# GLA attention fused with two MLPs on one core: the states' part of y in a bank of its own, the copy of k behind the sigmoid, and a new order of loads

## The chip, the cores and the metric

The kernel runs on one core of a Trainium2 chip. TensorE (PE) multiplies matrices and writes to PSUM, VectorE (DVE), ScalarE (ACT) and GpSimd (POOL) work on elements, SyncE (SP) only issues DMAs. Each engine works through its own instructions in the order in which they are written and waits at semaphores. The metric is the device time in microseconds of one execution. Times differ from run to run; a difference of 2% is what a measurement of this kernel can tell from no change.

## The reference, cut to what matters

```python
# attention: q, k, v, f_logit are (4, 8, 768, 48)
f = 1.0 / (1.0 + np.exp(-f_logit))
for t in range(S):
    state = f[:, :, t, :, None] * state + np.einsum('bhd,bhe->bhde', k[:, :, t], v[:, :, t])
    y[:, :, t] = np.einsum('bhd,bhde->bhe', q[:, :, t], state)
# x = y as (3072 tokens, 384)
gate = 1.0 / (1.0 + np.exp(-(x @ w_gate)))       # first MLP, d_ff 1536
x = gate * (x @ w_val) @ w_out
h = x @ w_in                                     # second MLP, d_ff 2048
out = (h * (1.0 / (1.0 + np.exp(-1.702 * h)))) @ w_out2
```

## The kernel before

**Attention.** A unit is a pair of heads and 256 tokens, 48 units in all, four to a step of 256 tokens (three steps to a batch, so that every third step begins with an empty state: `third` is 0). ACT turns f_logit into decays (`forget`, L545 and L546), DVE scans them (L722), takes the reciprocal (L726) and keeps the last value of each chunk (L727); the three together are `prepare`. POOL multiplies q and k by them (`decay`: q_dec L474, k_dec L479). The buffers f_raw, q_raw and k_raw have two slots, so that the loads for unit n must wait until unit n-2 was used: on SP, `load_kq(n)` waits for q_dec and then for k_dec of unit n-2.

**Visits.** PE does the matmuls of attention in 53 visits. The list `VISITS` says of each which unit is turned, kept and made; from the tenth on, visit n has (n, n-1, n-2). `turned`: two transposes of k_dec into the bank turn_ps (L914), which ACT copies to k_rows (`take_k`, L564), and the scores k_dec x q_dec (L957), which DVE masks (L734). `kept`: k_rows x v (L947), from which DVE makes four new states (L744, then a chain of three or four L752). `made`: scores x v (L935), and on top of these sums in the same columns the states times q_dec (L968), which make y. ACT copies y out (`take_y`, L570), and SP moves it by two or three small DMAs into x_raw, the input of the first MLP (`move_y`, L369).

**The MLPs.** Each product is made of three matmuls in a reduced format (L975 to L977: high x high, low x high, high x low), so that every operand is split into x_hi/x_lo, w_hi/w_lo and act_hi/act_lo. The first MLP goes through seven groups of tokens (two of 256, five of 512; here group 0 to 6) and in each through 12 blocks of hidden columns, j = 0 to 11. A block is on PE: 9 matmuls for the gate, 9 for the value (`hidden`), at some j a visit, then 9 matmuls of the block before into out_ps (`out`). ACT makes the sigmoid (L634) and act_hi (L640), DVE the product (L823) and act_lo (L832). The gate's matmuls of the next block wait for the sigmoid of this one, the value's for the product. Visits 0 to 7 run ahead of the MLP. Group 0 has visits at five blocks, groups 1 to 5 at j = 0, 1, 3, 4, 5, 7, 8 and 9. In group 0 DVE also splits the first MLP's weights (w_lo, L776), whose loads and high parts are ACT's (L520, L526).

**Where groups meet.** At j = 10 ACT makes the three slabs of x_hi for the next group (`x_first_part`, L584), and DVE then x_lo (L769). Slab k of x_hi needs the moved y of the first k+2 units of the next group's last step, so that the third slab needs the y that was made in this group's last visit, at j = 9. At j = 10 DVE also prepares the unit one further than the visit at j = 9 turned; PREPARE_AT sets this.

**SP's order.** For each visit SP issued the moves of y, v, then q and k for the unit three ahead, then f for the unit four ahead:

```python
if made is not None:
    move_y(made)
    load_v(made + 4)
if turned is not None:
    load_kq(turned + 3)
    load_f(turned + 4)
```

Of the kernel before, what the change touches and what calls it, by code (L numbers as in the profile page):

```python
# [12 lines left out]
P = 128  # L13
# [3 lines left out]
def gla_moe_moe2(nc, q_t, k_t, f_t, v_n, v_t, w1, w2, out_t, x_dram, x2_dram):  # L17
# [52 lines left out]
    for g in range(NG1 - 1):  # L70
        if g == 0:
            forgets = {j: n + 3 for n, j in enumerate((1, 2, 4, 6, 8))}
            prepares = {j: n + 1 for n, j in enumerate((0, 1, 3, 5, 7, 9))}
        else:
            forgets = {j: n + 3 for n, j in enumerate((0, 1, 3, 4, 5, 7, 8, 11))}
            prepares = {j: n + 2 for n, j in enumerate((0, 2, 3, 4, 6, 7, 10, 11))}
        FORGET_AT.update({(g, j): ahead_of + n for j, n in forgets.items()})
        PREPARE_AT.update({(g, j): ahead_of + n for j, n in prepares.items()})
        ahead_of += len(forgets)
# [4 lines left out]
    with ExitStack() as ctx:  # L84
# [40 lines left out]
        state = sb("state", [P, 2, UG, CH, D])  # L125
        p_end = sb("p_end", [P, UNITS, CH])
# [6 lines left out]

# [23 lines left out]
        tiles_done = sem("tiles_done")  # L157
# [4 lines left out]
        y_taken = sem("y_taken")  # L162
# [172 lines left out]
        with nc.Block() as block:  # L335

            @block.sync
            def _(sp):
# [25 lines left out]
                def move_y(n, pieces=slice(None)):  # L364
                    u = Unit(n)
                    sp.wait_ge(y_taken, n + 1)
# [36 lines left out]
                move_y(3, slice(1, None))  # L403
                for n in range(4, 8):
                    load_v(n)
# [4 lines left out]
                for q in range(BLOCKS1):  # L410
# [41 lines left out]
            def _(pool):  # L452
# [13 lines left out]
                def decay(n):  # L466
# [5 lines left out]
                    if n >= 4:  # L472
                        pool.wait_ge(visit_done, out_visit[n - 4] + 1)
# [41 lines left out]
            def _(act):  # L515
# [33 lines left out]
                def first_move_y(n, pieces):  # L549
                    u = Unit(n)  # L550
                    act.wait_ge(y_taken, n + 1)
# [52 lines left out]
                take_y(0)  # L604
# [4 lines left out]
                take_y(1)  # L609
                first_load_f(6)  # L610
                forget(5)
                w1_first_part(1)
                take_y(2)
                first_move_y(2, slice(2, None))
                take_y(3)
                first_move_y(3, slice(0, 1))
                first_load_f(7)
                load_w1(2)
                take_k(4)
                x_first_part(0)  # L620
                load_w1(3)
                w1_first_part(2)
                load_w1(4)
                forget(6)
                forget(7)

                for q, b in enumerate(BLOCK):
# [13 lines left out]
                    if b.first_mlp and (b.g, b.j) in VISIT_AT:  # L641
                        turned, _, made = VISITS[VISIT_AT[b.g, b.j]]
# [62 lines left out]
            def _(dve):  # L705
# [7 lines left out]
                for ps in (att_ps, out_ps):  # L713
                    dve.memset(ps[:, 0:2, Y_COL:Y_COL + BLOCKS * C], 0.0).then_inc(gaps_set, 1)

                def prepare(n):
                    if n >= UNITS:
                        return
# [4 lines left out]
                                           ALU.max).then_inc(scan_done, 1)  # L723
                    dve.wait_ge(scan_done, n + 1)
# [3 lines left out]
                                    prod[:, u.s, :].rearrange("p (c t) -> p c t", c=CH)[:, :, C - 1]).then_inc(p_end_done, 1)  # L728

# [368 lines left out]
```

## Time and profile before

| | |
|---|---|
| Time, three runs | 968.01, 969.16 and 1051.86 us; median 969.16 us |
| Profiled execution | 968.01 us, its span 966.2 us |
| Busy | PE 98%, PE's weight loads 82%, DVE 51%, ACT 31%, POOL 11% of the span |
| Chain that ended last | PE 90%, DVE 4%, waits without a cause shown 2%, DMA 1%, SP's queue 1%, ACT 1% |
| Granted PE clock | 0.99 on average; half (1.2 GHz instead of 2.4) in two stretches before 40 us |

The slowest of the three times is of a disturbed run and is left out of comparisons. Three stages follow one another: up to about 34 us attention's first visits and the first loads; up to about 480 us the first MLP with visits between its blocks (group 0 to 79.6 us, group 1 to 137 us); then MLP work without visits. The busy time of PE is that of pipelined instructions that overlap, so it does not say that PE never waited; the start times of neighbouring rows do.

### The profile page before, as it was taken

What the parts mean: (1) busy time and instruction counts of PE and PEld (TensorE: products, weight loads), DVE (VectorE), ACT (ScalarE), POOL (GpSimd) and SP (SyncE); (2) the same over time, 40 slices, a digit from 0 to 9 for tenths busy, and PEclk for the clock granted to TensorE, in tenths of its full rate; (3) what the DMA queues carried; (4) which work ended last, traced back from release to release, by engine and by line L of the source; (5) the groups of instructions that cost most, each with busy time, mean ns of one, the idle gap of its engine ahead of it and who ended that gap; (6) DMA issues with size and microseconds to landing.
All of it is one profiled execution on the core that took longest, in us unless ns stands there. A gap on an engine that the chain in (4) does not pass through costs nothing.

```text
span 966.2 us, 17729 instructions
## 1 busy us (share of the span) xinstructions
PE 948.8 (98%) x7159; PEld 789.7 (82%) x7159; DVE 491.9 (51%) x876; ACT 303.7 (31%) x621; POOL 106.9 (11%) x125
## 2 busy tenths in 40 slices
PE   8899999999999999999999999999999999999997
PEld 5799988888888888888788888888888888888886
DVE  8897876547555664565333234344343443443433
ACT  3453332223222222322224333323332233333322
POOL 4211211101110111111003440000000000000000
PEclk9899999999999999999999999999999999999999
DMA  5652322112111211121022330020020100100000
GB/s 152 204 167 61 83 63 67 53 51 66 52 46 42 82 45 50 33 76 28 24 104 66 98 115 1 0 66 1 1 66 1 55 12 1 66 1 1 33 1 35
DMA packets 44005, 52.33 MB, mean 54 GB/s; under 512 B 8464, under 2 KB 33808, under 8 KB 43920
## 3 DMA queue, kind: packets, MB, share of 16 engines
q1 hardware_dynamic: 41056, 43.20, 15.4%
q10 hardware_dynamic: 2864, 7.95, 2.8%
q8 instruction: 59, 0.97, 0.4%
q14 instruction: 26, 0.21, 0.1%
HBM read 36.96 MB, written 9.44 MB: 48 GB/s over the span
## 4 chain that ended last, share of the span: by engine, by line
PE 90%; DVE 4%; issue 2%; DMA 1%; SPq 1%; ACT 1%; ACTq 0%; POOL 0%; DVEq 0%
PE up_ps L975 16%; PE up_ps L977 16%; PE up_ps L976 16%; PE out_ps L975 12%; PE out_ps L977 11%; PE out_ps L976 11%; PE att_ps L968 3%; PE att_ps L935 2%; PE att_ps L957 1%; DMA stage<-w 1%; PE turn_ps L914 1%; PE att_ps L947 1%; DVE w_lo L776 1%; DMA k_raw<-k_t 1%; DVE act_lo L832 0%
## 5 line engine op out<-in xcount | busy, mean ns | idle before, releaser
L975 PE MATMUL up_ps<-x_hi,w_hi 128*128 128x512 f32 (+1 forms) x792 | 294.2, 372 | 3.6 <-ACT act_f L634 3.0
L977 PE MATMUL up_ps<-x_hi,w_lo 128*128 128x512 f32 (+1 forms) x792 | 293.8, 371 | 0.0
L976 PE MATMUL up_ps<-x_lo,w_hi 128*128 128x512 f32 (+1 forms) x792 | 293.7, 371 | 0.0
L975 PE MATMUL out_ps<-act_hi,w_hi 128*128 128x512 f32 (+1 forms) x540 | 207.9, 385 | 0.7 <-DVE act_lo L832 0.7
L977 PE MATMUL out_ps<-act_hi,w_lo 128*128 128x512 f32 (+1 forms) x540 | 202.9, 376 | 0.0
L976 PE MATMUL out_ps<-act_lo,w_hi 128*128 128x512 f32 (+1 forms) x540 | 202.6, 375 | 0.0
L640 ACT CAST act_hi<-act_f 128x512 fp32r<-128x512 f32 (+1 forms) x180 | 106.5, 592 | 253.0 <-DVE act_f L823 180.7
L832 DVE TENSOR_TENSOR act_lo<-act_f,act_hi 128x512 fp32r<-128x512 f32 (+1 forms) x180 | 118.1, 656 | 113.7 <-ACT act_hi L640 113.7
L975 PEld LDWEIGHTS up_ps<-x_hi,w_hi 128*128 128x128 f32 x792 | 150.0, 189 | 30.0 <-issue 3.6
L976 PEld LDWEIGHTS up_ps<-x_lo,w_hi 128*128 128x128 f32 x792 | 150.1, 190 | 25.3
L977 PEld LDWEIGHTS up_ps<-x_hi,w_lo 128*128 128x128 f32 x792 | 150.1, 189 | 25.2
L826 DVE TENSOR_TENSOR act_f<-act_f,up_ps 128x512 f32<-128x512 f32 x96 | 66.0, 687 | 173.4 <-ACT act_f L636 173.4
L823 DVE TENSOR_TENSOR act_f<-act_f,up_ps 128x512 f32<-128x512 f32 (+1 forms) x84 | 51.1, 608 | 163.0 <-PE up_ps L977 159.5
L975 PEld LDWEIGHTS out_ps<-act_hi,w_hi 128*128 128x128 f32 x540 | 101.6, 188 | 22.2 <-DVE act_lo L832 1.2
L636 ACT ACTIVATE act_f<-up_ps 128x512 f32<-128x512 f32 x96 | 57.4, 598 | 192.9 <-PE up_ps L977 192.9
L977 PEld LDWEIGHTS out_ps<-act_hi,w_lo 128*128 128x128 f32 x540 | 101.6, 188 | 18.7
L976 PEld LDWEIGHTS out_ps<-act_lo,w_hi 128*128 128x128 f32 x540 | 101.7, 188 | 17.3
L634 ACT ACTIVATE act_f<-up_ps 128x512 f32<-128x512 f32 (+1 forms) x84 | 45.0, 535 | 176.8 <-PE up_ps L977 176.8
L726 DVE RECIPROCAL inv_prod<-prod 128x256 f32<-128x256 f32 x48 | 84.1, 1753 | 1.7
L474 POOL TENSOR_TENSOR q_dec<-q_raw,prod 128x256 f32<-128x256 f32 x48 | 35.2, 734 | 317.5 <-DVE prod L722 263.6
L752 DVE SCALAR_TENSOR_TENSOR state<-state,p_end 128x48 f32<-128x48 f32 x176 | 47.4, 269 | 6.2
L479 POOL TENSOR_TENSOR k_dec<-k_raw,inv_prod 128x256 f32<-128x256 f32 x48 | 37.8, 788 | 50.1 <-issue 41.0
(68 smaller groups left out, 511.7 us busy)
## 6 DMA issues: line engine op xcount, KB each, us to landing
stage<-w SPq DMA_DIRECT2D x16, 384.0 KB, 3.2
stage<-w ACTq DMA_DIRECT2D x9, 576.0 KB, 4.4
q_raw<-q_t SPq DMA_DIRECT2D x96, 48.0 KB, 1.9
k_raw<-k_t SPq DMA_DIRECT2D x96, 48.0 KB, 1.9
v_raw<-v_n SPq DMA_DIRECT2D x48, 96.0 KB, 2.2
x_raw<-x_dram SPq DMA_DIRECT2D x6, 768.0 KB, 4.5
out_t<-final SPq DMA_DIRECT2D x18, 256.0 KB, 2.3
f_raw<-f_t SPq DMA_DIRECT2D x80, 48.0 KB, 1.9
```

The costliest lines, as they stand in the source:

```text
L479: pool.tensor_tensor(k_dec[:, u.s, :], k_raw[:, u.s, :], inv_prod[:, u.s, :], ALU.mult).then_inc(k_dec_done, 1)
L634: act.activation(act_f[:, b.t, 0:b.n], up_ps[:, 0, 0:b.n], ACT.Sigmoid).then_inc(sig_done, 1)
L636: act.activation(act_f[:, b.t, 0:b.n], up_ps[:, b.j % 2, 0:b.n], ACT.Sigmoid, scale=1.702).then_inc(sig_done, 1)
L640: act.copy(act_hi[:, b.t, 0:b.n], act_f[:, b.t, 0:b.n]).then_inc(act_hi_done, 1)
L726: dve.reciprocal(inv_prod[:, u.s, :], prod[:, u.s, :]).then_inc(inv_done, 1)
L752: dve.scalar_tensor_tensor(out=after[:, c, :], in0=state_before(u, c), scalar=p_end[:, n, c:c + 1], in1=after[:, c, :], op0=ALU.mult, op1= ...
L823: dve.tensor_tensor(act_f[:, b.t, 0:b.n], act_f[:, b.t, 0:b.n], up_ps[:, 1, 0:b.n], ALU.mult).then_inc(mul_done, 1)
L826: dve.tensor_tensor(act_f[:, b.t, 0:b.n], act_f[:, b.t, 0:b.n], up_ps[:, b.j % 2, 0:b.n], ALU.mult).then_inc(mul_done, 1)
L832: dve.tensor_tensor(act_lo[:, b.t, 0:b.n], act_f[:, b.t, 0:b.n], act_hi[:, b.t, 0:b.n].bitcast(F32), ALU.subtract).then_inc(act_split, 1)
L975: pe.matmul(dst, w_hi[:, at:at + P], m_hi, start=first, stop=False)
L976: pe.matmul(dst, w_hi[:, at:at + P], m_lo, start=False, stop=False)
L977: return pe.matmul(dst, w_lo[:, at:at + P], m_hi, start=False, stop=last)
```

## The change

It has five parts.

1. The states' part of y no longer adds to the columns of scores x v. `from_states` writes it into the upper half of turn_ps, behind the visit's other matmuls. ACT copies it to y_t (`begin_y`), and DVE adds the part from the visit's bank (`make_y`), which makes y. For a unit that begins with an empty state, `from_states` multiplies a zero tile for the first chunk too, two matmuls more.
2. Within the visit the wait for the visit's own earlier matmuls (`tiles_done`) is gone; there are waits for ACT's copy of the k just turned (`k_rows_done`) and for the y part before (`y_begun`) in front of it, since all three use the bank turn_ps.
3. ACT copies k to k_rows between sigmoid and act_hi instead of behind act_hi.
4. SP issues f, q and k for the units ahead in front of the moves of y and of v.
5. Ahead of the MLP the orders differ: ACT issues the loads of the first weights and makes their high parts at other places, `forget(7)` moves into block 0, DVE splits unit 4's `prepare` around two visits, and it now handles the visits 5 and 6 as well.

```diff
-            forgets = {j: n + 3 for n, j in enumerate((1, 2, 4, 6, 8))}
+            forgets = {j: n + 2 for n, j in enumerate((0, 1, 2, 4, 6, 8))}
@@ SP, at each visit
+                        if turned is not None:
+                            load_f(turned + 4)
+                            load_kq(turned + 3)
                         if made is not None:
                             move_y(made)
                             load_v(made + 4)
-                        if turned is not None:
-                            load_kq(turned + 3)
-                            load_f(turned + 4)
@@ POOL, decay
-                    if n >= 4:
-                        pool.wait_ge(visit_done, out_visit[n - 4] + 1)
+                    wait(pool, states_used, n - 3)
@@ ACT
-                def take_y(n):
-                    u = Unit(n)
-                    act.wait_ge(visit_done, out_visit[n] + 1)
+                def begin_y(n):
+                    act.wait_ge(states_used, n + 1)
                     wait(act, y_moved[n % YS], 16 * moves(n % YS, n))
-                    act.copy(y_t[:, n % YS, :].rearrange("p (c r t) -> p c r t", c=BLOCKS, r=SIDES),
-                             banks(out_visit[n])[:, :, Y_COL:Y_COL + BLOCKS * C].rearrange("p r (c t) -> p c r t", c=BLOCKS)).then_inc(y_taken, 1)
+                    act.copy(y_t[:, n % YS, :], turn_ps[:, W:2 * W]).then_inc(y_begun, 1)
@@ ACT, ahead of the blocks (after)
+                begin_y(1)
+                first_load_f(6)
+                load_w1(2)
+                forget(5)
+                begin_y(2)
+                first_move_y(2, slice(2, None))
+                w1_first_part(1)
+                begin_y(3)
+                first_move_y(3, slice(0, 1))
+                w1_first_part(2)
+                load_w1(3)
+                take_k(4)
+                x_first_part(0)
+                load_w1(4)
+                forget(6)
@@ ACT, in a block
+                    turned = made = None
+                    if b.first_mlp and (b.g, b.j) in VISIT_AT:
+                        turned, _, made = VISITS[VISIT_AT[b.g, b.j]]
+                    if turned is not None:
+                        take_k(turned)
                     act.wait_ge(mul_done, q + 1)
                     wait(act, act_used, q - 1)
                     act.copy(act_hi[:, b.t, 0:b.n], act_f[:, b.t, 0:b.n]).then_inc(act_hi_done, 1)
-                        if turned is not None:
-                            take_k(turned)
-                        if made is not None:
-                            take_y(made)
+                    if made is not None:
+                        begin_y(made)
@@ DVE
+                def make_y(n, v):
+                    dve.wait_ge(y_begun, n + 1)
+                    y = y_t[:, n % YS, :].rearrange("p (c r t) -> p r c t", c=BLOCKS, r=SIDES)
+                    own = banks(v)[:, :, Y_COL:Y_COL + BLOCKS * C].rearrange("p r (c t) -> p r c t", c=BLOCKS)
+                    dve.tensor_tensor(y, y, own, ALU.add).then_inc(y_done, 1)
@@ DVE, after_visit
-                    if made is not None:
-                        dve.wait_ge(y_taken, made + 1)
                     if turned is not None:
                         mask(turned, v)
                     if kept is not None:
                         new_states(kept, v)
+                    if made is not None:
+                        make_y(made, v)
@@ PE
+                def from_states(n, v):
+                    u = Unit(n)
+                    pe.wait_ge(state_done, states_before(n + 1))
+                    pe.wait_ge(k_rows_done, len([a for a, _, _ in VISITS[:v + 1] if a is not None]))
+                    wait(pe, y_begun, n)
+                    for c in range(CH):
+                        before = state_before(u, c) if u.third or c else no_state[:, :]
+                        for i in range(PAIR):
+                            last = pe.matmul(turn_ps[rows[i], W + c * C:W + (c + 1) * C], before[rows[i], :],
+                                             q_dec[rows[i], n % 4, c * C:(c + 1) * C], start=True, stop=True)
+                    last.then_inc(states_used, 1)
@@ PE, visit
+                    last.then_inc(visit_done, 1)
                     if made is not None:
-                        last.then_inc(tiles_done, 1)
-                        pe.wait_ge(tiles_done, made + 1)
-                        pe.wait_ge(state_done, states_before(made + 1))
-                        for c in range(0 if m.third else 1, CH):
-                            at = slice(Y_COL + c // SIDES * C, Y_COL + (c // SIDES + 1) * C)
-                            for i in range(PAIR):
-                                last = pe.matmul(ps[rows[i], c % SIDES, at], state_before(m, c)[rows[i], :],
-                                                 q_dec[rows[i], made % 4, c * C:(c + 1) * C], start=False, stop=False,
-                                                 skip_group_check=True)
-                    last.then_inc(visit_done, 1)
+                        from_states(made, v)
```

On SP, for the visit at j = 9 of group 1 (unit 15 made, unit 17 turned), before: two moves of y, v, q and k for unit 20, f for unit 21.

```order
L369 DMA x_raw<-y_t 48x256 [waits x_split,y_taken]
L369 DMA x_raw<-y_t 48x256
L361 DMA v_raw<-v_n 128x192 [waits visit_done]
L351 DMA q_raw<-q_t 48x256 [waits q_dec_done]
L351 DMA q_raw<-q_t 48x256
L354 DMA k_raw<-k_t 48x256 [waits k_dec_done]
L354 DMA k_raw<-k_t 48x256
L344 DMA f_raw<-f_t 48x256 [waits gate_done]
L344 DMA f_raw<-f_t 48x256
```

The same visit in the changed kernel: the two moves of y now stand behind the loads of q and k with their two waits.

```order
L345 DMA f_raw<-f_t 48x256 [waits gate_done]
L345 DMA f_raw<-f_t 48x256
L352 DMA q_raw<-q_t 48x256 [waits q_dec_done]
L352 DMA q_raw<-q_t 48x256
L355 DMA k_raw<-k_t 48x256 [waits k_dec_done]
L355 DMA k_raw<-k_t 48x256
L370 DMA x_raw<-y_t 48x256 [waits x_split,y_done]
L370 DMA x_raw<-y_t 48x256
L362 DMA v_raw<-v_n 128x192 [waits visit_done]
```

On PE, a visit of group 0 behind its transposes (block j = 2, unit 4 made), before.

```order
L957 MATMUL att_ps<-q_dec,k_dec 64x64 [waits q_dec_done]
L957 MATMUL att_ps<-q_dec,k_dec 64x64 x7
L968 MATMUL att_ps<-q_dec,state 48x64 [waits state_done,tiles_done]
L968 MATMUL att_ps<-q_dec,state 48x64 x7
```

The same place in the changed kernel: the eight matmuls of the states go to turn_ps, without the wait for the visit's own matmuls and with two others.

```order
L986 MATMUL att_ps<-q_dec,k_dec 64x64 [waits q_dec_done]
L986 MATMUL att_ps<-q_dec,k_dec 64x64 x7
L931 MATMUL turn_ps<-q_dec,state 48x64 [waits y_begun,k_rows_done,state_done]
L931 MATMUL turn_ps<-q_dec,state 48x64 x7
```

## Rows read from the trace of the kernel before

**Rows 1.** Busy time by stage (us, busy and count, PEclk, DMA share, GB/s).

```profile
34.00:79.60 45.60, 44.89 (x577) 42.73 (x577) 44.66 (x79) 21.26 (x48) 8.31 (x12) 0.93 0.54 157
79.60:137.00 57.40, 56.41 (x856) 53.11 (x857) 42.60 (x98) 20.22 (x62) 11.02 (x15) 1.00 0.28 74
```

**Rows 2.** The same view around the second stretch at half clock.

```profile
26.34:33.16 6.82, 4.41 (x46) 3.78 (x45) 3.79 (x7) 2.73 (x7) 2.99 (x4) 1.00 0.95 284
33.16:39.99 6.83, 5.90 (x53) 5.48 (x54) 5.97 (x8) 3.82 (x13) 1.46 (x2) 0.50 0.80 234
39.99:46.80 6.81, 6.72 (x107) 6.34 (x107) 6.64 (x13) 2.78 (x8) 1.47 (x2) 1.00 0.45 124
```

**Rows 3.** Who waited for whom (total us, times, longest): 138 to 480, DVE 34 to 79.6.

```profile
PEld att_ps L968 <- PE att_ps L957: 6.8, 30, 0.2
...
DVE act_f L823 <- ACT act_f L634: 2.0, 1, 2.0
```

**Rows 4.** Timeline of a visit in group 3, three chunks of states (start us, us).

```profile
238.05 0.38 PE L914 MATMUL turn_ps<-ident,k_dec 128*128 128x128 f32 x2
238.62 0.40 PE L947 MATMUL att_ps<-v_raw,k_rows 64*64 64x48 f32 x16
238.84 0.43 PE L957 MATMUL att_ps<-q_dec,k_dec 48*64 48x64 f32 x16
...
239.35 0.39 PEld L968 LDWEIGHTS att_ps<-q_dec,state 48*48 48x48 f32 x12 [0.23 <-PE att_ps L957]
...
239.82 0.19 PEld L975 LDWEIGHTS out_ps<-act_hi,w_hi 128*128 128x128 f32 x1
```

**Rows 5.** Timeline, weight loads of a visit with four chunks of states.

```profile
142.50 0.50 PEld L968 LDWEIGHTS att_ps<-q_dec,state 48*48 48x48 f32 x16 [0.23 <-PE att_ps L957]
143.09 0.19 PEld L975 LDWEIGHTS out_ps<-act_hi,w_hi 128*128 128x128 f32 x1
```

**Rows 6.** Timeline of the first visit: transposes and ACT's copy of k.

```profile
8.85 0.38 PE L914 MATMUL turn_ps<-ident,k_dec 128*128 128x128 f32 x2
...
9.27 0.37 ACT L564 COPY k_rows<-turn_ps 128x256 f32<-128x256 f32 x1 [3.40 <-PE turn_ps L914]
```

**Rows 7.** Timeline of DVE in group 0.

```profile
55.91 0.41 DVE L734 TENSOR_TENSOR scores<-att_ps,causal 128x256 f32<-128x256 f32 x1
...
56.24 0.34 DVE L744 TENSOR_TENSOR state<-att_ps,p_end 128x192 f32<-128x192 f32 x1
```

**Rows 8.** Timeline, end of the stage before the blocks.

```profile
31.72 1.15 ACT L526 CAST w_hi<-stage 128x1152 fp32r<-128x1152 f32 x1 [2.99 <-DMA stage<-w]
...
33.59 0.36 ACT L634 ACTIVATE act_f<-up_ps 128x256 f32<-128x256 f32 x1
...
33.98 0.42 DVE L823 TENSOR_TENSOR act_f<-act_f,up_ps 128x256 f32<-128x256 f32 x1 [2.01 <-ACT act_f L634]
```

**Rows 9.** Timeline of SP's queue, end of group 2.

```profile
212.01 1.98 SPq L369 DMA_DIRECT2D x_raw<-y_t  x2
...
223.72 0.78 SPq L354 DMA_DIRECT2D k_raw<-k_t  x2
```

**Rows 10.** Timeline of ACT and PE, end of group 2.

```profile
219.28 1.66 ACT L584 CAST x_hi<-x_raw 128x512 fp32r<-128x512 f32 x3
222.05 0.60 ACT L634 ACTIVATE act_f<-up_ps 128x512 f32<-128x512 f32 x1 [1.10 <-PE up_ps L977]
...
225.93 0.39 PE L975 MATMUL up_ps<-x_hi,w_hi 128*128 128x512 f32 x1
```

**Rows 11.** Timeline of SP's queue and PE, end of group 1.

```profile
137.06 0.78 SPq L354 DMA_DIRECT2D k_raw<-k_t  x2
...
136.59 0.47 PE L975 MATMUL up_ps<-x_hi,w_hi 128*128 128x512 f32 x1 [0.26 <-DVE x_lo L769]
...
137.63 0.49 PE L975 MATMUL up_ps<-x_hi,w_hi 128*128 128x512 f32 x1
```

**Rows 12.** DMA issues (count, KB each, median us to landing).

```profile
x_raw<-y_t SPq DMA_DIRECT2D x71, 48.0 KB, 2.0
```

More of the change, by code:

```diff
@@ L78, in gla_moe_moe2 @@
         PREPARE_AT.update({(g, j): ahead_of + n for j, n in prepares.items()})
-        ahead_of += len(forgets)
+        ahead_of += 5 if g == 0 else 8
     SPLIT_AT1 = 10
@@ L125, in gla_moe_moe2 @@
         state = sb("state", [P, 2, UG, CH, D])
+        no_state = sb("no_state", [P, D])
         p_end = sb("p_end", [P, UNITS, CH])
@@ L156, in gla_moe_moe2 @@
         k_rows_done = sem("k_rows_done")
-        tiles_done = sem("tiles_done")
         visit_done = sem("visit_done")
@@ L161, in gla_moe_moe2 @@
         state_done = sem("state_done")
-        y_taken = sem("y_taken")
+        states_used = sem("states_used")
+        y_begun = sem("y_begun")
+        y_done = sem("y_done")
         y_moved = sems("y_moved", YS)
@@ L365, in move_y @@
                     u = Unit(n)
-                    sp.wait_ge(y_taken, n + 1)
+                    sp.wait_ge(y_done, n + 1)
                     wait(sp, x_split, u.group * KC)
@@ L403, in _ @@
                 move_y(3, slice(1, None))
+                load_f(7)
                 for n in range(4, 8):
@@ L550, in first_move_y @@
                     u = Unit(n)
-                    act.wait_ge(y_taken, n + 1)
+                    act.wait_ge(y_done, n + 1)
                     for src, slab, dst in pieces_of_pair(u.p)[pieces]:
@@ L603, in _ @@
                 first_load_f(5)
-                take_y(0)
+                begin_y(0)
                 w1_first_part(0)
@@ L640, in _ @@
                     act.copy(act_hi[:, b.t, 0:b.n], act_f[:, b.t, 0:b.n]).then_inc(act_hi_done, 1)
-                    if b.first_mlp and (b.g, b.j) in VISIT_AT:
-                        turned, _, made = VISITS[VISIT_AT[b.g, b.j]]
-                        if turned is not None:
-                            take_k(turned)
-                        if made is not None:
-                            take_y(made)
+                    if made is not None:
+                        begin_y(made)
                     if b.first_mlp and (b.g, b.j) in FORGET_AT:
@@ L711, in _, with begin_decay @@
                 dve.memset(floor[:, :, :], SAFE_PRODUCT).then_inc(gaps_set, 1)
[L713 to L718, printed above, removed]
+                for ps in (att_ps[:, 0:2, Y_COL:Y_COL + BLOCKS * C], out_ps[:, 0:2, Y_COL:Y_COL + BLOCKS * C], turn_ps[:, W:2 * W]):
+                    dve.memset(ps, 0.0).then_inc(gaps_set, 1)
+                dve.memset(no_state[:, :], 0.0).then_inc(gaps_set, 1)
+                def begin_decay(n):
                     u = Unit(n)
@@ L723, in prepare, with end_decay @@
                                            ALU.max).then_inc(scan_done, 1)
+                def end_decay(n):
+                    u = Unit(n)
                     dve.wait_ge(scan_done, n + 1)
@@ L728, in prepare @@
                                     prod[:, u.s, :].rearrange("p (c t) -> p c t", c=CH)[:, :, C - 1]).then_inc(p_end_done, 1)
+                def prepare(n):
+                    if n < UNITS:
+                        begin_decay(n)
+                        end_decay(n)
+                def make_y(n, v):
[3 more added lines that the diff above has]
+                    dve.tensor_tensor(y, y, own, ALU.add).then_inc(y_done, 1)
                 def mask(n, v):
@@ L801, in flag @@
                     dve.tensor_scalar(unsafe[0:1, 0:1], least[0:1, 0:1], -1.0, 1.0, ALU.mult, ALU.add).then_inc(flag_done, 1)
-                dve.wait_ge(gaps_set, 7)
+                dve.wait_ge(gaps_set, 9)
                 prepare(0)
@@ L810, in _ @@
                 after_visit(2)
+                begin_decay(4)
                 after_visit(3)
                 after_visit(4)
-                prepare(4)
+                end_decay(4)
+                after_visit(5)
+                after_visit(6)
                 w1_second_part(1)
@@ L904, in _ @@
                 pe.wait_ge(consts_set, CONSTS)
+                def from_states(n, v):
+                    u = Unit(n)
+                    pe.wait_ge(state_done, states_before(n + 1))
[7 more added lines that the diff above has]
+                    last.then_inc(states_used, 1)
                 def visit(v):
@@ L911, in visit @@
                         wait(pe, k_rows_done, turned)
+                        wait(pe, y_begun, len([c for _, _, c in VISITS[:v] if c is not None]))
                         for c in range(BLOCKS):
@@ L924, in visit @@
                         if before[2] is not None:
-                            pe.wait_ge(y_taken, before[2] + 1)
+                            pe.wait_ge(y_done, before[2] + 1)
                     opens = True
                     if made is not None:
-                        m = Unit(made)
                         pe.wait_ge(scores_masked, made + 1)
```

9 lines of the change are left out of this document (removed).

## The prediction

> **What bounds the kernel now.** I read the page first: PE is busy 98% of the span and stands for 90% of the chain that ended last, so a change is worth what it takes from or adds to PE's own row of instructions, or what it makes PE wait. Then busy time by stage [rows 1]. In group 1 (79.6 to 137 us) PE is full and DVE busy 42.6 of 57.4 us, with gaps. In group 0 DVE is as full as PE: 44.66 of 45.60 us, and in the view of waits DVE waits for one thing there only, 2.0 us at the very start [rows 3]. So from 34 to 79.6 us DVE sets the pace, and what DVE gets on top comes out of the time one to one; behind that PE sets it. The reader should then look at a visit [rows 4]: PE's own drain is a gap in it, counted as 6.8 us over 30 visits [rows 3].
>
> **The drain inside a visit.** From the k x v part to the scores is 238.84 - 238.62 = 0.22 us, and from the scores to the states 239.35 - 238.84 = 0.51 us [rows 4]. Without the drain the states would follow as the other parts do, so 0.29 us goes. 44 visits between blocks make y; four lie in group 0, where DVE sets the pace and a faster PE gains nothing. That leaves 40 x 0.29 = **-11.6 us**. What is late next is ACT's copy of k, for which PE now waits there. In the first visit it began 9.27 - 8.85 = 0.42 us behind the transposes' start and took 0.37 [rows 6], so it ends 0.79 us behind it; with some 0.1 us for the signal 0.9. PE reaches the states 0.22 us behind 238.84, that is 1.01 us behind the transposes at 238.05 [rows 4]. So the copy is just in time, by 0.1 us, if ACT is free, and it is: the copy now stands behind the sigmoid, which is ready a whole part of the block earlier. Bounds: 0.29 saved, or 0.1 if the copy's signal is late by 0.2; I take 0.29, since the margin is positive in the rows.
>
> **Two matmuls more for units that begin empty.** Three chunks of states take 239.82 - 239.35 = 0.47 us to the next weight load, four 143.09 - 142.50 = 0.59 [rows 4, 5]. 12 units made outside group 0 begin a batch: 12 x 0.12 = **+1.4 us**. That the matmuls write one bank instead of alternating costs nothing that a row shows; the parts with four quadrants busy run at 0.22 us into either bank.
>
> **make_y on DVE.** It reads PSUM and writes 128x256, as the mask does, which costs 56.24 - 55.91 = 0.33 us from start to start [rows 7]. In group 0 four of them are paid in full: **+1.3 us**. In group 1 they fall into DVE's gaps, and DVE no longer waits for ACT's copy ahead of the mask; in the later groups DVE is busy little over half the time. I take 0 there, at most 1 us where two visits follow in consecutive blocks of 256 tokens.
>
> **Ahead of the blocks.** The third weights' load is issued some 6 us earlier, so that its high part no longer makes the first sigmoid wait (the cast at 31.72 stands in front of 33.59 [rows 8]). But DVE gets the additions for units 2 and 3, and ACT waits for each before it moves y. Walked through by durations, x_hi comes about 2 us later, DVE then splits x, prepares unit 5 (about 2.4 us) and masks, and comes to its first product at about 33.8 us instead of 33.98 [rows 8]. PE's stall shrinks, DVE's start doesn't move. **0**, between -1.5 and +2.
>
> **The moves of y behind the loads.** Within a group nothing is late: the units that the loads wait for were prepared a block or more before. At j = 9 it is different. `load_kq(turned + 3)` waits for k_dec of a unit that DVE prepares only at j = 10; the row shows it, k's DMAs issued at 223.72 while y's moves had gone at 212.01 [rows 9]. In the changed order y's two moves stand behind, so that they start at 223.72 + 0.78 = 224.5, the second at about 225.1, and it lands 2.0 us later [rows 12] at 227.1. The third slab of x_hi, which was made from 219.28 on [rows 10], needs exactly that unit. It ends at about 227.7 (1.66 / 3 = 0.6 us each). ACT's queue holds the sigmoid of block 11 behind it, 222.05 before, now 227.75 to 228.35, and PE's next gate waits for that sigmoid. PE stood ready at 225.93 [rows 10]; it starts at 228.4 or, with a slower landing, 229. I take 2.7 us, between 2.3 and 3.4. Groups 2, 3 and 4 end so; group 5 doesn't, since its last visits turn nothing: 3 x 2.7 = 8.1. At the end of group 1 k goes at 137.06 [rows 11], so the same steps give 140.4 for the landing, 141.0 for x_hi, 141.5 for PE. PE started at 136.59 and lost another 0.3 before 137.63 [rows 11]: 4.6 us. Together **+12.7 us**.
>
> **PE's clock.** Between 26.34 and 33.16 us PE was busy 4.41 of 6.82 us, and then ran a stretch of 6.83 us at half clock, 53 matmuls instead of the 107 of the next [rows 2]. Such a stretch costs 3.4 us where PE sets the pace. The new waits are of the size of the idle time in front of that stretch (2.4 us): 2.7 us three times and some 5 us once. Smaller gaps, 0.3 to 0.5 us near 137 us [rows 11], left the clock full. So a fall is likely at each, not sure: I take three of four, 3 x 3.4 = **+10.2 us**, between 0 and 13.6. The Trainium skill speaks against it: "TensorE: Matmul & The Clock Gate", section "HAM oscillation — how this bites in real kernels", puts the loss down to waits longer than those three and counts shorter gaps as harmless. By it only the long wait would cost clock. The row before the fall at 33.16, with 2.4 us of idle time, doesn't bear the rule out.
>
> **The sum.** -11.6 + 1.4 + 1.3 + 0 + 12.7 + 10.2 = +14.0 us against the profiled execution's 968.0, or 982.0. The median of the runs is 1.2 us above it, so **983 us**, 1.4% slower. 2% of the median, 19.4 us, is what a measurement of this kernel can tell from no change: 949.8 and 988.5 are the limits.
>
> **Rivals.**
> *The clock holds at the short waits.* For it: no row shows how a single wait of 2.7 us between full blocks acts, and the stages before 40 us had other gaps too. Then one fall at most: -11.6 + 1.4 + 1.3 + 12.7 + 3.4 = +7.2, 976 us, or 973 with none.
> *The moves of y are not late enough to matter*, for instance because x_hi's third slab isn't the last thing that PE waits for. Against it: ACT's queue is strictly in order, and every step above has its row. Then -11.6 + 2.7 = -8.9: 960 us.
> *The copy of k takes the drain's place*, and the kernel is slower beyond the limit. PE would wait at the states for k_rows instead of for itself. It decides from a signal that comes 0.1 us later than I reckon: at 0.4 us later nothing of the 11.6 us is left, and ACT's copy sits in front of act_hi, which then moves too. 983 + 11.6 = 995 us; with half of it 989. For it: the margin is only 0.1 us. Against it: ACT has nothing else to do there.
> *The change doesn't do what it says*: the drain goes but PE waits for DVE, because the pace in group 1 turns to DVE as well (42.6 us of 57.4, plus 8 x 0.33). This costs at most 3 us and stays inside the range.
>
> **How the numbers follow.** Stalls with most of the clock falls 0.48 (977 to 990 us, most likely 983); stalls, the clock mostly holding, 0.22 (971 to 979); no stalls 0.12 (958 to 964); the copy of k in the way 0.13 (987 to 996); the rest 0.05. The range of 8 in 10 leaves out the third case and the end of the fourth: 970 to 992. Slower than 988.5 is most of the fourth case and the upper end of the first: 0.17. Faster by 2% needs -19 us, which nothing here offers: 0.01. Within 2%: 0.82.
>
> **What the changed kernel's profile would show.** The drain: weight loads of the states 0.22 us behind those of the scores, no wait of PE for itself in a visit, or else one for ACT's k_rows. Group 0: DVE without gaps, its end some 1.3 us later. The moves: at the end of groups 1 to 4 an ACT wait for x_raw by DMA, SP's moves behind k, and a PE wait for act_f of 2.3 to 3.4 us, 4 to 5 at the first; group 5 without. The clock: half for a stretch of some 7 us behind most of these waits. The prediction is wrong if x_hi's third slab isn't late, if the visits don't get shorter, or if the clock stays full throughout.

## The result, and the profile after

The changed kernel took 977.79 us (median; 977.04 to 978.27), the one before 969.58: a ratio of 1.0088, 95% interval 1.0074 to 1.0102. It is 0.9% slower, by 8.2 us, clear of the noise but far below 2%. One of the six executions before, 1051.86 us, was a disturbed one: without it the median is 969.16 us, and the ratio is taken without it. The profiled execution of the changed kernel took 978.27 us with a span of 976.5; the span before was 966.2, so the traces have 10.3 us to account for.

The states' part of y, in a visit of group 3 (timeline of PE after and, last, ACT's copy of k; start us, us):

```profile
245.43 0.38 PE L944 MATMUL turn_ps<-ident,k_dec 128*128 128x128 f32 x2
...
246.00 0.40 PE L976 MATMUL att_ps<-v_raw,k_rows 64*64 64x48 f32 x16
246.22 0.43 PE L986 MATMUL att_ps<-q_dec,k_dec 48*64 48x64 f32 x16
246.47 0.29 PE L931 MATMUL turn_ps<-q_dec,no_state 48*48 48x64 f32 x4
246.58 0.52 PE L931 MATMUL turn_ps<-q_dec,state 48*48 48x64 f32 x12
247.03 0.50 PE L995 MATMUL out_ps<-act_hi,w_hi 128*128 128x512 f32 x1
...
245.85 0.37 ACT L565 COPY k_rows<-turn_ps 128x256 f32<-128x256 f32 x1 [1.67 <-PE turn_ps L944]
```

A visit with four chunks of states before (timeline of PE):

```profile
141.20 0.38 PE L914 MATMUL turn_ps<-ident,k_dec 128*128 128x128 f32 x2
...
143.09 0.38 PE L975 MATMUL out_ps<-act_hi,w_hi 128*128 128x256 f32 x1
```

The states now begin 1.04 us behind the transposes, where they began 1.30 behind them [rows 4], and the block's output follows at +1.60. It followed at +1.89 in a visit with four chunks of states and at +1.78 in one with three, so 28 visits became 0.29 us shorter and 12 became 0.18 us shorter: -10.3 us. PE waits for ACT's copy of k in none of them; the copy ends at +0.79, 0.25 us before the states begin.

What came instead stands where groups meet. The waits after (total us, times, longest):

```profile
ACT x_hi L583 <- DMA x_raw<-y_t: 19.9, 3, 6.8
...
PE up_ps L995 <- ACT act_f L631: 11.9, 4, 5.1
...
ACT x_hi L583 <- issue: 6.8, 1, 6.8
```

Four times, at the ends of groups 1 to 4, ACT waits for a moved y, and PE for ACT's sigmoid. PE's rows and the sigmoids behind them put the first wait at 4.8 us and the others at 2.6 each, 12.6 in all; the 11.9 us of the view of waits are the idle time alone. The end of group 2, from SP's, ACT's and PE's timelines:

```profile
228.65 0.78 SPq L355 DMA_DIRECT2D k_raw<-k_t  x2
229.52 1.16 SPq L370 DMA_DIRECT2D x_raw<-y_t  x2
...
224.21 1.14 ACT L583 CAST x_hi<-x_raw 128x512 fp32r<-128x512 f32 x2
232.14 0.62 ACT L583 CAST x_hi<-x_raw 128x512 fp32r<-128x512 f32 x1 [6.79 <-DMA x_raw<-y_t]
232.66 0.59 ACT L631 ACTIVATE act_f<-up_ps 128x512 f32<-128x512 f32 x1
...
230.63 0.39 PE L997 MATMUL out_ps<-act_hi,w_lo 128*128 128x512 f32 x1
233.30 0.50 PE L995 MATMUL up_ps<-x_hi,w_hi 128*128 128x512 f32 x1 [2.29 <-ACT act_f L631]
```

Before, the three slabs of x_hi came in one piece and PE went on without a gap [rows 10]. Now the third slab waits 6.8 us for its y, whose moves stand in SP's queue behind k. The sigmoid that frees PE stands in ACT's queue behind the slab.

The clock around these waits, by stretches (us, busy and count, PEclk, DMA share, GB/s):

```profile
140.25:147.05 6.80, 5.54 (x13) 4.39 (x14) 3.82 (x6) 2.32 (x6) 1.46 (x2) 0.50 0.16 44
324.55:327.95 3.40, 3.40 (x10) 2.64 (x9) 2.96 (x3) 1.39 (x4) 0.73 (x1) 0.50 0.10 29
416.65:420.05 3.40, 3.40 (x10) 2.69 (x9) 3.07 (x4) 1.03 (x4) 0.86 (x2) 0.51 0.17 43
```

It fell at three of the four waits, not at that of group 2. At the end of group 1 it fell while PE still waited (PE's next matmul starts at 141.51), at the ends of groups 3 and 4 when PE had been running again for 1.1 and 1.5 us. But two of the stretches at half clock are 3.4 us long, half the one seen before [rows 2], and in the long one PE was idle for 1.3 us. Half of what is left is the cost: (6.8 - 1.3 + 3.4 + 3.4) / 2 = 6.2 us.

In front of the blocks (ACT and DVE):

```profile
28.85 1.15 ACT L527 CAST w_hi<-stage 128x1152 fp32r<-128x1152 f32 x1 [1.12 <-DVE y_t L741]
...
32.53 0.38 ACT L631 ACTIVATE act_f<-up_ps 128x256 f32<-128x256 f32 x1 [0.64 <-PE up_ps L997]
...
34.44 0.41 DVE L839 TENSOR_TENSOR act_f<-act_f,up_ps 128x256 f32<-128x256 f32 x1
```

The sigmoid comes 1.1 us earlier than before, DVE's product 0.46 us later [rows 8]; from there to the first sigmoid of group 1 another 1.5 us are lost. The sum is 0.5 + 1.5 - 10.3 + 12.6 (the waits) + 6.2 (the clock) = +10.5, against the 10.3 us.

### The profile page after: what moved, and what is told of

It is laid out like the page before. It is cut to its first block, busy times and chain, and to the rows that moved or that the text cites. A ratio compares the mean times of both kernels' runs of the same rounds, so it can differ in the third digit from the quotient of the medians.

```text
span 976.5 us, 17865 instructions
## 1 busy us (share of the span) xinstructions
PE 948.2 (97%) x7223; PEld 791.4 (81%) x7223; DVE 505.5 (52%) x926; ACT 307.2 (31%) x621; POOL 106.2 (11%) x125
## 4 chain that ended last, share of the span: by engine, by line
PE 57%; DVE 0%; DMA 0%; ACT 0%; SPq 0%; issue 0%; ACTq 0%
PE up_ps L995 10%; PE up_ps L997 10%; PE up_ps L996 10%; PE out_ps L995 9%; PE out_ps L997 8%; PE out_ps L996 8%; PE turn_ps L931 0%; PE att_ps L964 0%; DMA x_raw<-y_t 0%; PE att_ps L976 0%; PE att_ps L986 0%; PE turn_ps L944 0%; SPq L355 0%; DVE act_lo L848 0%; DVE act_f L842 0%
## 5 line engine op out<-in xcount | busy, mean ns | idle before, releaser
L995 PE MATMUL up_ps<-x_hi,w_hi 128*128 128x512 f32 (+1 forms) x792 | 296.9, 375 | 13.9 <-ACT act_f L631 11.9
L475 POOL TENSOR_TENSOR q_dec<-q_raw,prod 128x256 f32<-128x256 f32 x48 | 35.2, 734 | 328.1 <-DVE prod L719 247.6
```

The costliest lines, as they stand in the source:

```text
L995: pe.matmul(dst, w_hi[:, at:at + P], m_hi, start=first, stop=False)
```

## The experiments

Each kernel was timed in five rounds beside the kernel before, which gave 968.9 to 969.1 us. L numbers differ by a few from kernel to kernel.

### SP's old order everywhere, and at one visit of each group

The changed kernel with the old order on SP:

```diff
+                        if made is not None:
+                            move_y(made)
+                            load_v(made + 4)
                         if turned is not None:
-                            load_f(turned + 4)
                             load_kq(turned + 3)
-                        if made is not None:
-                            move_y(made)
-                            load_v(made + 4)
+                            load_f(turned + 4)
```

> The kernel after, with the old order on SP at every visit: the moves of y and of v stand ahead of the loads for units ahead. Theory: the four waits at the ends of groups 1 to 4 (12.6 us together in the trace after) come from the moves that are issued behind the loads, and the half-speed stretches behind three of them (about 6 us) come with them, so both go: 978 - 12.6 - 6 = about 960 us; the loads now stand behind a wait for make_y, which in groups 0 and 1 is late (DVE is packed there), so up to 6 us may come back there: 960 to 966. Rival: the waits are DVE's late make_y or the landing of the moves in themselves, whatever the order: 978 unchanged.

The changed kernel with the moves in front at j = 9 alone:

```diff
+                        moves_first = b.j == 9
+                        if made is not None and moves_first:
+                            move_y(made)
+                            load_v(made + 4)
                         if turned is not None:
                             load_f(turned + 4)
                             load_kq(turned + 3)
-                        if made is not None:
+                        if made is not None and not moves_first:
```

> The kernel after, with the moves of y and v ahead of the loads at one visit of each group only, the tenth (j = 9), the last whose moves the next MLP block waits for. Theory (the order at that one visit makes the waits): 969.6 + 0.5 (first sigmoid) + 1.4 (DVE in group 0) - 10.3 (shorter visits) = 961 us, and no wait of PE for act_f at the ends of groups 1 to 4 over 1 us. If the loads of the other visits matter too, e1 is faster than this one by over 1 us. Rival (waits independent of the order): 978.

Measured: 960.37 us for the second (ratio 0.9914, 0.9901 to 0.9928), and 969.78 for the first (1.0008). The one place, j = 9, is worth 17.4 us of the changed kernel. The end of group 2 in the second, ACT's timeline:

```profile
217.09 1.66 ACT L587 CAST x_hi<-x_raw 128x512 fp32r<-128x512 f32 x3
219.85 0.60 ACT L635 ACTIVATE act_f<-up_ps 128x512 f32<-128x512 f32 x1 [1.10 <-PE up_ps L1001]
```

The row of three slabs is back, as in [rows 10], and no wait for act_f is left at a group's end. The sum in the expectation came out within a microsecond.

The first kernel missed its range, by 4 us. The waits at the ends went there too, but it lost 9.4 us elsewhere, and all of it early: its sigmoids are 2.0 us behind those of the second kernel at the start of group 1, 9.3 at its tenth block and 9.6 at the start of group 2, and equal in pace from there on. The reason, from ACT's waits between 34 and 84 us and between 84 and 140 us, and then from ACT's and SP's timelines in group 1:

```profile
ACT gate L546 <- DMA f_raw<-f_t: 7.0, 4, 2.7
ACT gate L546 <- DMA f_raw<-f_t: 16.2, 5, 4.3
```

```profile
98.40 0.41 ACT L546 ACTIVATE gate<-f_raw 128x252 f32<-128x252 f32 x1 [2.33 <-DMA f_raw<-f_t]
98.72 0.19 ACT L547 ACTIVATE floor<-f_raw 128x4 f32<-128x4 f32 x1
98.82 0.36 ACT L631 ACTIVATE act_f<-up_ps 128x256 f32<-128x256 f32 x1
...
98.50 1.80 SPq L370 DMA_DIRECT2D x_raw<-y_t  x3
...
102.84 1.65 SPq L345 DMA_DIRECT2D f_raw<-f_t  x2
```

SP sends the move only when make_y, the last of DVE's steps in a visit, is done (it starts at 97.98 and the move at 98.50), and f stands at the end of what follows. ACT's next gate waits for that f with the sigmoid behind it, 23.2 us in all up to 140 us, where the second kernel has 2.5. Some of the 9.4 us can be the clock's and not the waits': this kernel's trace has 13.7 us at half clock and the second's 6.8, which is worth 3.4 us at most. So the new order isn't idle: once y is finished on DVE, loads in front of moves are worth 9.4 us in groups 0 and 1. The prediction had looked at the new order's costs only.

### The moves in front in all later visits

```diff
-                        moves_first = b.j == 9
+                        moves_first = b.j == 9 or b.g >= 2
```

> The kernel with the moves first at j = 9, with the moves first at every visit of groups 2 to 5 as well. Theory (the loads in front of the moves are needed only where make_y is late, in groups 0 and 1; the 9.6 us that the old order cost at all visits were lost in those two groups): 960.4, within 1. Rival (the loads' place matters in the later groups too): above 961.5; or, if the early moves help there, below 959.5.

Measured: 960.9 us (0.9919, 0.9906 to 0.9933), no difference from 960.4. In groups 2 to 5 the order matters at j = 9 and nowhere else.

### The new order alone

The kernel before, with only the loads in front of the moves:

```diff
+                        if turned is not None:
+                            load_f(turned + 4)
+                            load_kq(turned + 3)
                         if made is not None:
                             move_y(made)
                             load_v(made + 4)
-                        if turned is not None:
-                            load_kq(turned + 3)
-                            load_f(turned + 4)
```

> The kernel before with nothing but the new order on SP: the loads for units ahead are issued in front of the moves of y and v. Theory: the waits at the ends of groups 1 to 4 appear in full, with their half-speed stretches: 969.6 + 12.6 + 6 = 988 us (985 to 991), less if the early loads give something back in group 1 (up to 3 us). Rival (the waits need the other parts of the change, such as the later make_y or the k copy on ScalarE): 970 to 975.

Measured: 984.9 us (1.0163, 1.0149 to 1.0177), +15.9 us, just under the expected 985 to 991. The waits of that kernel:

```profile
ACT x_hi L584 <- DMA x_raw<-y_t: 20.0, 3, 6.8
PE up_ps L975 <- ACT act_f L634: 13.7, 5, 5.1
```

They are the same waits with the same lengths, so they need neither make_y on DVE nor the k copy's place. The clock fell at two of them here, for 6.8 us at the end of group 1 and for 3.4 at the end of group 2, and stayed full at the ends of groups 3 and 4, where it had fallen in the changed kernel.

### Is the clock's part real?

The changed kernel, with PE kept busy where it would wait:

```diff
+                        if b.j == 0 and 2 <= b.g <= 5:
+                            seen = VISITS[:VISIT_AT[b.g - 1, 9] + 1]
+                            pe.wait_ge(k_rows_done, len([a for a, _, _ in seen if a is not None]))
+                            pe.wait_ge(y_begun, len([c for _, _, c in seen if c is not None]))
+                            for _ in range(20 if b.g == 2 else 10):
+                                pe.matmul(turn_ps[:, 0:P], ident[:, :], ident[:, :], start=True, stop=True)
                         wait(pe, sig_done, q)
```

> The kernel after, with matmuls of 128 x 128 by the identity put into a spare part of the transposes' bank ahead of PE's wait for the sigmoid of the first visit of groups 2 to 5 (20 for group 2, 10 each for the others), so that PE is busy in the time in which it would wait; the results are not used. Theory: the half-speed stretches come from the idle time, and busy work in it takes them away: 978 - 6 = 972 us, with a granted clock of 0.99 or more through the blocks of groups 2 to 5. Rival (the clock falls for another reason, or costs nothing): 978. If the extra matmuls stand in the way of the block instead of in its wait: 979 to 982.

Measured: 976.41 us, 1.4 us below the kernel after and not 6. By its total this comes near the rival, so the stretches have to be read one by one. The end of group 3, PE's timeline and the windows:

```profile
322.30 2.39 PE L1037 MATMUL turn_ps<-ident 128*128 128x128 f32 x20
325.40 0.50 PE L995 MATMUL up_ps<-x_hi,w_hi 128*128 128x512 f32 x1 [0.70 <-ACT act_f L631]
...
326.89 0.39 PE L995 MATMUL up_ps<-x_hi,w_hi 128*128 128x512 f32 x1
```

```profile
324.55:327.95 3.40, 2.70 (x13) 2.14 (x12) 2.38 (x4) 2.01 (x6) 0.00 (x0) 1.00 0.00 0
44.50:51.50 7.00, 6.50 (x43) 6.39 (x44) 5.50 (x12) 2.91 (x8) 0.88 (x2) 0.53 0.60 197
```

Most of the idle time is filled, and the clock stays full at all four waits. From the first gate matmul behind the wait to the tenth sigmoid of the next group this kernel takes 2.6, 0.0, 1.6 and 1.6 us less than the kernel after, for the ends of groups 1, 2, 3 and 4: 5.8 us, near the 6.2 counted from the stretches, and nothing at the one end where the clock hadn't fallen. The kernel with the moves in front at j = 9 runs the same stretches 2.2, 0.1, 1.8 and 1.7 us faster than the kernel after, which is 5.8 us too. Two things ate the gain. The waits themselves became longer, by 3.3 us together, since the moves landed later (in the view of DMA issues 2.5 us for 1.9 around 320 us; at the end of group 1 SP also took 2.4 us instead of 1.2 to issue them). And a stretch at half clock at 44.3 us lasted 6.8 us and not 3.4, for 1.8 us more by the tenth block of group 1. That one is far ahead of the edit. Why the moves were slower, I can't say: the extra matmuls touch no transfer.

### Where the k copy stands

The kernel with the moves in front at j = 9, with `take_k` back behind act_hi:

```diff
-                    if turned is not None:
-                        take_k(turned)
                     act.wait_ge(mul_done, q + 1)
                     wait(act, act_used, q - 1)
                     act.copy(act_hi[:, b.t, 0:b.n], act_f[:, b.t, 0:b.n]).then_inc(act_hi_done, 1)
+                    if turned is not None:
+                        take_k(turned)
```

> The kernel with the moves first at j = 9, with the k copy put back behind the act_hi copy on ScalarE. Theory: PE's matmuls from the states wait for the k copy, since both use the transposes' bank. In a visit of group 2 the states begin 1.04 us after the transposes and the k copy, which starts at +0.42 now, would start only when act_hi has been issued, at +1.64, and end at +2.0: about 1.0 us of waiting for each of the 40 visits with a transpose, 960 + 38 = 998 us (990 to 1005). Rival (the copy is hidden at either place, so that this part of the change is worth nothing): 960 to 962.

Measured: 1003.11 us (1.0348, 1.0331 to 1.0364), 42.7 us above the 960.4 of the kernel that it changes. A visit of that kernel, PE's timeline:

```profile
249.78 0.38 PE L948 MATMUL turn_ps<-ident,k_dec 128*128 128x128 f32 x2
...
251.76 0.32 PE L935 MATMUL turn_ps<-q_dec,no_state 48*48 48x64 f32 x4 [0.76 <-issue]
```

The states begin 1.98 us behind the transposes, not 1.04. By its sigmoids this kernel loses 35.2 of the 42.7 us behind the start of group 1, where its clock stays full: that is the visits alone, most of them 0.94 us longer each. The other 7.6 us are lost in group 0, where four waits in front of the states (7.6 us against 1.1) and more half clock (20.5 us up to 63 us, against 6.8) stand together; no run separates them. With the new order, the move of the states into the transposes' bank is a gain only with the copy at its new place.

### DVE's pace

The kernel with the moves in front at j = 9, with one reduction more on DVE behind each make_y, in group 0 (shown) or in groups 2 to 5:

```diff
+                        if b.g == 0 and VISITS[v][2] is not None:
+                            dve.tensor_reduce(spare_y[:, :], causal[:, :].unsqueeze(1).to_broadcast([P, 16, C]), AX_X, ALU.add)
```

> The kernel with the moves first at j = 9, with one reduction of 1024 elements (about 1.0 to 1.1 us, not used) more on DVE behind each make_y in the four visits of group 0 that have one. Theory (DVE sets the pace of group 0): each costs its whole duration, 960.4 + 4.3 = 964.7 us, and make_y's own 4 x 0.33 stands in the time at the same rate. Rival (DVE's work in group 0 is hidden as elsewhere): 960 to 961.

> The same reduction on DVE behind each make_y, in the visits of groups 2 to 5 only (some 28 of them, 29 us of work in all). Theory (DVE is behind PE there and has the time): 960.4 unchanged, at most +1. Rival (make_y and what follows it delays the next visit's or block's inputs): up to +29, 989 us.

Measured: 965.0 us (+4.6) with four of them in group 0, and 960.9 with 32 in the later groups, which is no difference. The two views of that tile (ns, minimum, median and maximum):

```profile
L860 DVE TENSOR_REDUCE spare_y<-causal x4: 1214/1215/1216, 49.6 to 79.9; 128x16 f32<-128x1024 f32 x4
```

```profile
L860 DVE TENSOR_REDUCE spare_y<-causal x32: 1209/1213/1216, 147.3 to 474.0; 128x16 f32<-128x1024 f32 x32
```

4 x 1.21 = 4.9 us of work cost 4.6 us in group 0, and 39 us of the same work cost nothing in groups 2 to 5. The 4.6 may hold some of the clock: the traces of both kernels have 13.7 us at half clock before 52 us, where the kernel without reductions has 6.8. Between these two traces, alike in this, the four reductions make 3.0 us at the first sigmoid of group 1. So most of DVE's work in group 0 is paid for, between 3.0 and 4.6 of 4.9 us; group 1 was not tested.

### The weights' order alone

The kernel before, with three steps of ACT's list in other places:

```diff
                 first_load_f(6)
+                load_w1(2)
                 forget(5)
-                w1_first_part(1)
                 take_y(2)
                 first_move_y(2, slice(2, None))
+                w1_first_part(1)
                 take_y(3)
                 first_move_y(3, slice(0, 1))
                 first_load_f(7)
-                load_w1(2)
+                w1_first_part(2)
+                load_w1(3)
                 take_k(4)
                 x_first_part(0)
-                load_w1(3)
-                w1_first_part(2)
                 load_w1(4)
```

> The kernel before with nothing but the new order of the first weights on ScalarE: the load of the third piece of w1 ahead of the sixth gate, its first split ahead of the last w1 load, the split of the second behind the third y. Theory: the first sigmoid comes up to 1.1 us earlier (32.5 for 33.6), and DVE, which waited for it, starts its first product up to 1 us earlier: 969.0 - 1 = 968.0 us (967 to 969). Rival (DVE or the weights' landing sets the first product): 969.0. Rival (the later split of the second piece holds the second block): 970.

Measured: 967.46 us (0.9988, 0.9979 to 0.9997), -1.6 us, a little more than the 1 us expected and within its range. The first sigmoid and the first product there:

```profile
31.14 0.36 ACT L634 ACTIVATE act_f<-up_ps 128x256 f32<-128x256 f32 x1
```

```profile
32.67 0.41 DVE L823 TENSOR_TENSOR act_f<-act_f,up_ps 128x256 f32<-128x256 f32 x1
```

The product comes 1.3 us earlier than in the kernel before. In the full change it comes 0.46 us later, so that the rest of the change in front of the blocks takes about 1.8 us. DVE's additions, and ACT's wait of 1.12 us for one of them in the rows after, point to them; no run has them alone.

### Relieving DVE in group 0

If DVE sets the pace there, GpSimd could take some of its work. Four pieces of the weights' low part go to it (in a second kernel two), on top of the moves in front at j = 9 (not shown: DVE leaves these pieces out, and PE waits for w1_pool too):

```diff
                 for n in range(7, UNITS):
                     decay(n)
+                    if n - 7 < len(ON_POOL):        # ON_POOL = (5, 7, 9, 11), or (5, 9)
+                        t = ON_POOL[n - 7]
+                        piece = slice(t * PIECE1, (t + 1) * PIECE1)
+                        pool.wait_ge(w1_hi_done, t + 1)
+                        pool.tensor_tensor(w_lo[:, piece], w1_staged(t), w_hi[:, piece].bitcast(F32),
+                                           ALU.subtract).then_inc(w1_pool, 1)
```

> The kernel with the moves first at j = 9, with the second half (w_lo) of four pieces of w1, the 6th, 8th, 10th and 12th, made on GpSimd instead of on DVE during group 0. Theory (DVE sets the pace of group 0, as the runs with more work on it showed): DVE has 4 x 1.35 = 5.4 us less to do; PE alone would need about 49.5 us for group 0 where it takes 52.6, by the blocks and visits of group 1, so about 3 us are to be had: 960.4 - 3 = 957.4 us (955 to 958.5). Rival: GpSimd's subtraction (estimated at 2.6 us for 1152 columns, from 1.13 us for 384 and 1.84 us for 768 in the trace) comes too late for PE or makes DVE's own work slower: 960 to 963.

> The same with two pieces on GpSimd, the 6th and the 10th. Theory: DVE has 2.7 us less, and the time falls by about as much while DVE sets the pace: 958 us (957.5 to 959). Rival (as above): 960 to 962.

Measured: 965.78 us with four and 963.64 with two, against 960.4: slower by 5.4 and 3.3. The rival won, by more than its 960 to 963 and 960 to 962. GpSimd and DVE with four pieces:

```profile
58.54 2.68 POOL L529 TENSOR_TENSOR w_lo<-final,w_hi 128x1152 fp32r<-128x1152 f32 x1 [1.71 <-ACT w_hi L546]
```

```profile
58.64 0.34 DVE L776 TENSOR_TENSOR state<-att_ps,p_end 128x192 f32<-128x192 f32 x1
59.01 3.18 DVE L784 SCALAR_TENSOR_TENSOR state<-state,p_end 128x48 f32<-128x48 f32 x4
62.11 0.41 DVE L760 TENSOR_TENSOR y_t<-y_t,att_ps 128x256 f32<-128x256 f32 x1
```

and DVE without:

```profile
57.47 1.18 DVE L769 SCALAR_TENSOR_TENSOR state<-state,p_end 128x48 f32<-128x48 f32 x4
```

The four state updates take 3.18 us instead of 1.18, and 3.1 to 3.2 us in all four visits that GpSimd's pieces meet; asked for that stretch alone, the view gives 2.27 us to the first of them, which ends when GpSimd's subtraction does, at 61.2. So each piece costs DVE 2.0 us. It gives back 0.7 only, since the piece had stood in time in which DVE otherwise waits for ACT's act_hi (product to act_lo 0.88 us without it, 1.60 with it). 4 x 1.3 = 5.2 us of the 5.4, and the half clock in this kernel's trace is that of the kernel without pieces. With two pieces it would be 2.6 of the 3.3; that trace has 17.1 us at half clock before 80 us instead of 6.8, which can be the rest.

## Why the prediction was right

The time was forecast as 983 us within 970 to 992; it is 977.8.

**The drain.** Right in mechanism and size: -11.6 + 1.4 = -10.2 forecast, -10.3 read from the visits. The margin for the k copy, 0.1 us by my reckoning, held: the rival in which the copy takes the drain's place has no row in the trace after, and the copy ended 0.25 us before the states began. The 0.1 us for the signal in that reckoning has no row of its own. The run with the copy moved back is not this rival, which had the copy late by its signal alone: there act_hi stands in front of the copy, and the two together cost 42.7 us. That rival's price of 12 us was not tested.

**make_y on DVE.** Forecast +1.3 in group 0 and none later; group 0 became 1.5 us longer, with all that changed in it (forget(7) moved into it too, and it had 3.4 us at half clock where it had 6.8), so make_y's own part is not measured. The runs with extra work on DVE bear out the rule behind it: most of the work counts in group 0 and none from group 2 on.

**Ahead of the blocks.** Forecast 0 between -1.5 and +2; read +0.46. The zero was two things, as the run of the order alone shows: the first product 1.3 us earlier by the order, and 1.8 later by the rest.

**The moves behind the loads.** Right. 12.7 us forecast and 12.6 read, 4.8 at the end of group 1 and 2.6 at each of the next three, none at the end of group 5. The run with nothing but the moves put back at j = 9 removed them, and the run with nothing but the new order made them. What the step lacked is that the same order gives something: with y finished late on DVE, it saves 9.4 us in groups 0 and 1. That didn't enter the sum because the sum never asked what the other parts of the change would cost with the old order.

**PE's clock.** This is the term that was mis-sized: 10.2 us forecast, three falls of 3.4 us each; three falls came, and they cost 6.2 by the stretches, 5.8 by the run without idle time. The number of falls was right, in part by luck: the same four waits in the run of the new order alone brought two. Two stretches were 3.4 us long, half as long as the one in the trace before on which I had priced them, and 1.3 us of the long one was idle time of PE, which costs nothing a second time. The rule of the Trainium skill ("TensorE: Matmul & The Clock Gate", section "HAM oscillation — how this bites in real kernels"), which would count only the longer wait, fits one fall of the three: with waits of 2.6 us the clock fell at the ends of groups 3 and 4 and stayed full at the end of group 2. The rival that the clock holds at the short waits, 976 us, was off in its cause and within 2 us in its time, because the falls cost so little.

Of the 5.2 us between forecast and median, 3.7 lie between the profiled executions (982.0 forecast, 978.3 measured), where the clock's term was 4.0 too high and the others together a little low. The rest comes from the profiled executions themselves: the one before lay 1.2 us under its median, the one after 0.5 above.

## What to carry to other kernels

When a queue's order is changed, look for the one place in each period where the item that was moved back is the last thing somebody needs, and leave the old order there: here one condition, j = 9, turned 0.9% slower into 0.9% faster. Ask of an order also what it protects: the old one at every visit cost 9.4 us more than at j = 9 alone, since another part of the change had made its first item late. And when work goes to an idle engine, check whether the busy engine can run while it does.

## What the runs showed of the hardware

A subtraction of 128x1152 on GpSimd, 2.68 us, held up a DVE instruction with two operands in SBUF to its end (2.27 us for one that takes 0.3), while one that reads PSUM, at 58.64, ran in its usual 0.34 us. The Trainium skill states this as a rule, in "SBUF — State Buffer", section "SBUF: two separate sides": the two engines share a pair of ports, held for a whole instruction. The trace agrees.

Stretches of PE at half clock came in three lengths: 3.4 and 6.8 us in most kernels, and 10.2 us before 30 us in the trace with the copy of k moved back and in the one with two pieces on GpSimd. At the end of group 1, with a wait of 5.1 us, it was 6.8 us, and with the waits of 2.6 us it was 3.4; before 50 us the kernel before had two of 6.8 us [one of them in rows 2] and the kernel after two of 3.4. The same wait of 2.6 us between full blocks brought one at the ends of groups 3 and 4 and none at the end of group 2 in the kernel after; with the new order alone it brought one at the end of group 2 and none at the other two. So the length of the wait alone doesn't decide it, and what does stays open. So does the slower landing of the moves, 2.5 us for 1.9, in the run with extra matmuls.
